# Where the buffers of a fused convolution and two-layer MLP kernel begin: TensorE's streamed operands on 2048-byte boundaries

## The chip, the cores and the metric

The kernel runs on one core of one Trainium2 chip. The time is the device time of one execution in microseconds (us). The kernel before took 1140.1 us, the median of 3 runs (1139.94 to 1140.52).

## What is computed

The input x has 2 sequences of 4096 tokens with 192 channels. Three steps follow, all in float32 in the reference:

```python
# 1. causal convolution: 7 taps, a softmax of 8 heads' weights, 24 channels to a head
out[b, s, h, :] = sum_k w[h, k] * x_pad[b, s + k, h, :]
# 2. a first MLP, 192 -> 2048 -> 192, leaky
h = x @ w_in;  g = np.maximum(0.01 * h, h);  y = g @ w_out
# 3. a second MLP of the same size, smooth
h = y @ w_in2; g = h if h >= 1, 0 if h <= -1, else (h + 1)**2 / 4;  z = g @ w_out2
```

## The kernel before

The 8192 tokens are cut into 16 tiles of T = 512 tokens. Channels lie on the 128 partitions and tokens along the free dimension; the 192 channels are split into a main part of 128 and an edge part of 64. A job is one layer for one tile, so there are 32 jobs; leaky and smooth jobs of neighbouring tiles alternate.

A job goes through CHUNKS = 16 chunks of 128 hidden channels. For each chunk, TensorE makes `hidden` from the tile's operands and the weights w_main and w_edge; ScalarE and VectorE apply the activation and write `g`; the second matmuls add `g` times w_out to `acc_main` and `acc_edge`. To keep float32's precision, each value that TensorE streams is split into a rounded part (`hi`) and the rest (`lo`), both of type fp32r, and so are the weights. ScalarE makes g_hi from g (L682), VectorE makes g_lo = g - g_hi (L951). All streamed operands of the two layers are such buffers of 512 fp32r elements per partition, 2048 bytes: op_hi, op_lo, op_edge and op_top (for both layers, two each: 16 buffers) and g_hi and g_lo (SLOTS = 4 each: 8 buffers).

TensorE's order is written out by hand. Each matmul uses 64 of the array's 128 rows: `top_first` and `top_second` issue for the upper half (partitions 0 to 63), `bottom_first` and `bottom_second` for the lower half. `two_chunks` interleaves them so that one matmul of each half runs beside one of the other: 38 matmuls, 19 for each half, per two chunks. Only the last 20 matmuls (`whole_edge`, `whole_main`) use all 128 rows. In the opening, 16 small matmuls (`keep_warm`, L615) and an edge convolution (L622), both in plain f32, go ahead; the convolution streams 256 elements of x_edge0.

Lines that the prediction speaks of: L411, L413, L415 and L417 are the upper half's matmuls for `hidden`, L429 to L445 the lower half's; L472 to L485 are the upper half's second matmuls, L501 to L513 the lower half's. L522 to L536 are the whole-array ones.

The order in which `sb(...)` is called sets each buffer's address: one buffer is laid behind the other in the partition's memory, each rounded up to 32 bytes. In the kernel before, the weights come first, then the stages for loading weights, ten small buffers for the taps' softmax and `taps`, the x buffers, the op buffers, conv, pre and g, g_hi and g_lo, and the result's buffers. The small tap buffers are written and read once, in the opening.

Of the kernel before, what the change touches and what calls it, by code (L numbers as in the profile page):

```python
# [9 lines left out]

# [1 line left out]

# [4 lines left out]
F32R = mybir.dt.float32r  # L19
# [3 lines left out]

P = 128
T = 512
Q = 32
GROUPS = T // Q
AHEAD = 3
# [4 lines left out]
SLOTS = 4  # L33
# [14 lines left out]
def bass_conv_mlp_mlp(nc, x, weight, moe_w_in, moe_w_out, moe2_w_in, moe2_w_out, out):  # L48
    B, S, D = x.shape
    H, TAPS = weight.shape  # L50
    F = moe_w_in.shape[1]
    GROUP = D // H
    HALO = TAPS - 1
    EDGE = D - P
    CHUNKS = F // P
    HALF = T // 2
    TILES = B * S // T
    STORES = D // Q
    LOADS = P // Q
    assert LOADS == 2 * EDGE // Q  # L60
    PIECES = 8
    PC = CHUNKS // PIECES
    PW = PC * P
# [3 lines left out]

    x_rows = x.rearrange("b s d -> (b s) d").rearrange("(g r) d -> r g d", r=Q)
    out_rows = out.rearrange("(g r) d -> r g d", r=Q)
    w_in_dram = (moe_w_in, moe2_w_in)  # L70
    w_out_dram = tuple(w.rearrange("(c p) d -> p c d", p=P) for w in (moe_w_out, moe2_w_out))

    with ExitStack() as ctx:
        def sb(name, shape, dt=F32):
            return ctx.enter_context(nc.sbuf_tensor(name, shape, dt))

        def psum(name):
            return ctx.enter_context(nc.psum_tensor(name, [P, T], F32))

# [5 lines left out]
        w_main = [sb(f"w_main{l}", [P, 2, F], F32R) for l in (0, 1)]  # L85
        w_edge = [sb(f"w_edge{l}", [P, 2, F], F32R) for l in (0, 1)]
        w_out = [sb(f"w_out{l}", [P, CHUNKS, 2 * D], F32R) for l in (0, 1)]

        stage = [sb(f"stage{i}", [P, 2 * PW + PC * D]) for i in range(AHEAD)]

        taps_raw = sb("taps_raw", [P, H, TAPS])
        taps_max = sb("taps_max", [P, H])
        taps_sub = sb("taps_sub", [P, H, TAPS])
        taps_exp = sb("taps_exp", [P, H, TAPS])
        taps_sum = sb("taps_sum", [P, H])
        taps_den = sb("taps_den", [P, H])
        taps_inv = sb("taps_inv", [P, H])
        own = sb("own", [P, 3, H])
        own_inv = sb("own_inv", [P, 2, H])
        own_taps = sb("own_taps", [P, 2, H, TAPS])  # L100
        taps = sb("taps", [P, 2, TAPS])

        x_in = [sb(f"x_in{b}", [P, T]) for b in (0, 1)]
        x_in_edge = [sb(f"x_in_edge{b}", [P, HALF]) for b in (0, 1)]
        x_main = [sb(f"x_main{b}", [P, HALO + T]) for b in (0, 1)]
        x_edge = [sb(f"x_edge{b}", [P, HALO + HALF]) for b in (0, 1)]

        op_hi = [[sb(f"op_hi{l}{b}", [P, T], F32R) for b in (0, 1)] for l in (0, 1)]
        op_lo = [[sb(f"op_lo{l}{b}", [P, T], F32R) for b in (0, 1)] for l in (0, 1)]
        op_edge = [[sb(f"op_edge{l}{b}", [P, T], F32R) for b in (0, 1)] for l in (0, 1)]
        op_top = [[sb(f"op_top{l}{b}", [P, T], F32R) for b in (0, 1)] for l in (0, 1)]
        conv_main = sb("conv_main", [P, T])
        conv_edge = sb("conv_edge", [P, HALF])

        pre = [sb(f"pre{i}", [P, T]) for i in (0, 1)]
        g = [sb(f"g{i}", [P, T]) for i in range(SLOTS)]
        g_hi = [sb(f"g_hi{i}", [P, T], F32R) for i in range(SLOTS)]  # L120
        g_lo = [sb(f"g_lo{i}", [P, T], F32R) for i in range(SLOTS)]

        edge_b = sb("edge_b", [EDGE, T])
        edge_sum = sb("edge_sum", [EDGE, T])
        y_main = sb("y_main", [P, T])
        y_edge = sb("y_edge", [EDGE, T])

        hidden = [psum(f"hidden{i}") for i in range(SLOTS)]
        acc_main = [psum(f"acc_main{i}") for i in (0, 1)]
# [986 lines left out]
```

How the kernel before makes its waits and increments, by code:

```python
        @block.sync  # L273
# [29 lines left out]
            def store(t, b, pos):  # L303
                group = b * (S // Q) + pos * GROUPS
                sp.wait_ge(y_main_ready, t + 1)
                for q in range(D // Q):
                    if q == P // Q:
                        sp.wait_ge(y_edge_ready, t + 1)
                    src = y_main[Q * q:Q * (q + 1), :] if q < P // Q else y_edge[Q * q - P:Q * (q + 1) - P, :]
                    sp.dma_start(out_rows[:, bass.ds(group, GROUPS), Q * q:Q * (q + 1)],
                                 src.rearrange("r (g c) -> r g c", c=Q)).then_inc(stored, 16)
            load_x_main(EVEN, 0, parts=P // Q - 1)
            load_x_edge(EVEN, 0, parts=range(2))
            load_weights(1)
            load_x_main(ODD, 0)
            load_weights(2)
            load_x_edge(ODD, 0)
            for piece in range(AHEAD, 2 * PIECES):
                sp.wait_ge(stage_used, piece - AHEAD + 1)
                load_weights(piece)
                if piece == PIECES:
                    sp.wait_ge(x_turned, 2)
                    load_x(EVEN, 1)
            with sp.Fori(0, PASSES) as j:
                sp.wait_ge(x_turned, 4 * j + 4)
                load_x(ODD, j + 1)
                store(2 * j, EVEN, j)
                sp.wait_ge(x_turned, 4 * j + 6)
# [1 line left out]
                store(2 * j + 1, ODD, j)  # L331
            store(TILES - 2, EVEN, TILES // 2 - 1)
            sp.wait_ge(y_edge_ready, TILES)
            for q in range(P // Q, D // Q):
```

## Time and profile before

| | before |
|---|---|
| median of 3 runs | 1140.1 us |
| profiled execution's own time | 1139.77 us |
| its span, first to last instruction | 1138.0 us |
| PE busy | 1126.9 us (99%), 9754 matmuls |
| VectorE (DVE) busy | 897.3 us (79%) |
| ScalarE (ACT) busy | 797.8 us (70%) |
| mean granted TensorE clock | 0.999 of full speed |

The span is the time between the first and the last instruction of the profiled execution; the device time is slightly longer. "Busy" of an engine is the time covered by at least one of its instructions; PE is the matmuls and PEld the weight loads, which run beside them. A matmul's duration in the profile is modelled and longer than its distance to the next one, because matmuls overlap in the array; the distance between starts is what can be counted on.

### The profile page before, as it was taken

Reading aid. Unit: us, or ns where it says so; the run is one execution under the profiler, and the core shown is the slowest. Engines: PE = TensorE matmul, PEld = TensorE weight load, DVE = VectorE, ACT = ScalarE, POOL = GpSimd, SP = SyncE. Lnnn points to the kernel's source line nnn. Section 1 sums busy time; section 2 is a strip of 40 time slices with the busy share of each in tenths; the row PEclk is TensorE's granted clock in tenths of the full one; section 3 lists DMA queues with packets and bytes.
Section 4 is the critical chain, followed back from the end, with each engine's and each line's share of the span. In section 5 each row is a group of like instructions: output and inputs, shape, how many; then the busy total and the mean of one; then the engine's idle time right before and its main releaser. Section 6 shows DMA issues by size and latency. Waiting matters only on the chain.

```text
span 1138.0 us, 25723 instructions
## 1 busy us (share of the span) xinstructions
PE 1126.9 (99%) x9754; PEld 922.7 (81%) x9754; DVE 897.3 (79%) x1511; ACT 797.8 (70%) x1472; POOL 50.3 (4%) x76
## 2 busy tenths in 40 slices
PE   7999999999999999999999999999999999999998
PEld 6788888888888888888888888888888888888886
DVE  7787877888777887788877788787787877888665
ACT  6768767586775867758577685866758667686685
POOL 5533000000000000000000000000000000000000
PEclk9999999999999999999999999999999999999999
DMA  6330000101001010010100101001010100100001
GB/s 142 97 80 2 14 16 1 29 2 25 5 1 30 1 29 1 1 29 1 29 1 8 23 1 29 1 13 18 1 29 1 24 7 1 29 1 15 1 1 28
DMA packets 114569, 21.98 MB, mean 19 GB/s; under 512 B 106257, under 2 KB 114449, under 8 KB 114449
## 3 DMA queue, kind: packets, MB, share of 16 engines
q1 hardware_dynamic: 111600, 19.61, 9.4%
q8 instruction: 77, 1.26, 0.5%
q10 hardware_dynamic: 2848, 0.75, 0.3%
q14 instruction: 44, 0.35, 0.1%
HBM read 14.05 MB, written 6.29 MB: 18 GB/s over the span
## 4 chain that ended last, share of the span: by engine, by line
PE 93%; DVE 3%; ACT 2%; issue 1%; DMA 0%; DVEq 0%; ACTq 0%
PE hidden L417 14%; PE acc_edge L475 10%; PE acc_main L481 10%; PE acc_main L483 10%; PE acc_main L485 10%; PE hidden L413 10%; PE hidden L415 10%; PE hidden L411 10%; PE acc_edge L472 10%; DVE g_lo L951 1%; DVE g L940 0%; ACT g_hi L682 0%; DVE acc_main L887 0%; ACT pre L670 0%; DVE acc_main L851 0%
## 5 line engine op out<-in xcount | busy, mean ns | idle before, releaser
L682 ACT CAST g_hi<-g 128x512 fp32r<-128x512 f32 x510 | 299.2, 618 | 280.2 <-PE acc_main L513 214.4
L951 DVE TENSOR_TENSOR g_lo<-g,g_hi 128x512 fp32r<-128x512 f32 x510 | 335.0, 690 | 104.1 <-ACT g_hi L682 99.3
L945 DVE SCALAR_TENSOR_TENSOR g<-hidden,pre 128x512 f32<-128x512 f32 x256 | 176.7, 690 | 105.9 <-ACT pre L670 100.5
L417 PE MATMUL hidden<-op_edge,w_edge 64*128 64x512 f32 x768 | 257.3, 388 | 0.0
L411 PE MATMUL hidden<-op_hi,w_main 64*128 64x512 f32 x512 | 198.9, 389 | 3.2 <-DVE g L940 1.7
L429 PE MATMUL hidden<-op_hi,w_main 64*128 64x512 f32 x512 | 199.2, 389 | 0.0
L433 PE MATMUL hidden<-op_hi,w_main 64*128 64x512 f32 x512 | 198.9, 388 | 0.0
L413 PE MATMUL hidden<-op_lo,w_main 64*128 64x512 f32 x512 | 198.8, 388 | 0.0
L438 PE MATMUL hidden<-op_edge,w_edge 64*128 64x512 f32 x512 | 198.7, 388 | 0.0
L431 PE MATMUL hidden<-op_lo,w_main 64*128 64x512 f32 x512 | 198.7, 388 | 0.0
L415 PE MATMUL hidden<-op_hi,w_main 64*128 64x512 f32 x512 | 198.7, 388 | 0.0
L475 PE MATMUL acc_edge<-g_lo,w_out 64*128 64x512 f32 x508 | 197.6, 389 | 0.5 <-DVE g_lo L951 0.5
L501 PE MATMUL acc_edge<-g_hi,w_out 64*128 64x512 f32 x508 | 197.2, 388 | 0.0
L472 PE MATMUL acc_edge<-g_hi,w_out 64*128 64x512 f32 x508 | 197.1, 388 | 0.0
L509 PE MATMUL acc_main<-g_hi,w_out 64*128 64x512 f32 x508 | 197.1, 388 | 0.0
L513 PE MATMUL acc_main<-g_lo,w_out 64*128 64x512 f32 x508 | 197.1, 388 | 0.0
L481 PE MATMUL acc_main<-g_hi,w_out 64*128 64x512 f32 x508 | 197.1, 388 | 0.0
L485 PE MATMUL acc_main<-g_lo,w_out 64*128 64x512 f32 x508 | 197.1, 388 | 0.0
L511 PE MATMUL acc_main<-g_hi,w_out 64*128 64x512 f32 x508 | 197.1, 388 | 0.0
L483 PE MATMUL acc_main<-g_hi,w_out 64*128 64x512 f32 x508 | 197.1, 388 | 0.0
L503 PE MATMUL acc_edge<-g_lo,w_out 64*128 64x512 f32 x508 | 197.1, 388 | 0.0
L940 DVE SCALAR_TENSOR_TENSOR g<-hidden,pre 128x512 f32<-128x512 f32 x256 | 172.5, 680 | 17.5 <-ACT pre L663 13.9
(128 smaller groups left out, 2778.2 us busy)
## 6 DMA issues: line engine op xcount, KB each, us to landing
x_in<-in_x_dram SPq DMA_DIRECT2D x67, 64.0 KB, 2.3
out_dram<-y_main SPq DMA_DIRECT2D x62, 64.0 KB, 1.8
stage<-in_moe_w_out_dram SPq DMA_DIRECT2D x15, 192.0 KB, 2.7
x_in_edge<-in_x_dram SPq DMA_DIRECT2D x66, 32.0 KB, 1.9
out_dram<-y_edge SPq DMA_DIRECT2D x32, 64.0 KB, 1.8
stage<-in_moe_w_in_dram SPq DMA_DIRECT2D x15, 128.0 KB, 2.3
stage<-in_moe_w_in_dram SPq DMA_DIRECT2D x30, 64.0 KB, 2.3
stage<-in_moe_w_out_dram ACTq DMA_DIRECT2D x1, 192.0 KB, 4.0
```

The lines of the kernel that those rows point to most:

```text
L411: nc.tensor.matmul(h[:], w_main[l][top, 0, cols], op_hi[l][b][top, :], start=True, stop=False)
L413: nc.tensor.matmul(h[:], w_main[l][top, 0, cols], op_lo[l][b][top, :], start=False, stop=False)
L415: nc.tensor.matmul(h[:], w_main[l][top, 1, cols], op_hi[l][b][top, :], start=False, stop=False)
L417: done = nc.tensor.matmul(h[:], w_edge[l][top, i - 3, cols], op_edge[l][b][top, :], start=False, stop=False)
L429: nc.tensor.matmul(h[:], w_main[l][bottom, 0, cols], op_hi[l][b][bottom, :], start=False, stop=False)
L472: nc.tensor.matmul(edge[:], w[:, P:2 * P], hi, start=k == 0, stop=False)
L475: done = nc.tensor.matmul(edge[:], w[:, P:2 * P], lo, start=False, stop=False)
L481: nc.tensor.matmul(main[:], w[:, 0:P], hi, start=k == 0, stop=False)
L483: nc.tensor.matmul(main[:], w[:, 2 * P:], hi, start=False, stop=False)
L485: done = nc.tensor.matmul(main[:], w[:, 0:P], lo, start=False, stop=False)
L682: nc.scalar.copy(hi_of(n, c)[:], g[c % SLOTS][:]).then_inc(g_hi_ready, 1)
L951: nc.vector.tensor_tensor(lo_of(n, c)[:], g[c % SLOTS][:], hi_of(n, c)[:].bitcast(F32), ALU.subtract).then_inc(g_lo_ready, 1)
```

## The change

The order of the buffers is altered, and a filler is put in. Weights stay where they are. Behind them come `taps`, x_edge0 and the filler `to_line`, whose size is computed from the first free byte (16,512) and the weights' 114,688 bytes, so that the op buffers, g_hi and g_lo begin on multiples of 2048 bytes. Stages and x buffers move behind them. The ten small tap buffers are no longer buffers of their own: they are parts of y_main. The instructions, their order, the semaphores and the waits are the same.

```diff
+LINE = 2048
+FIRST_FREE = 16512
...
-        stage = [sb(f"stage{i}", [P, 2 * PW + PC * D]) for i in range(AHEAD)]
-        taps_raw = sb("taps_raw", [P, H, TAPS])
-        taps_max = sb("taps_max", [P, H])
...
         taps = sb("taps", [P, 2, TAPS])
-        x_in = [sb(f"x_in{b}", [P, T]) for b in (0, 1)]
-        x_in_edge = [sb(f"x_in_edge{b}", [P, HALF]) for b in (0, 1)]
-        x_main = [sb(f"x_main{b}", [P, HALO + T]) for b in (0, 1)]
-        x_edge = [sb(f"x_edge{b}", [P, HALO + HALF]) for b in (0, 1)]
+        x_edge = [sb("x_edge0", [P, HALO + HALF])]
+        sb("to_line", [P, (LINE - (FIRST_FREE + 114688) % LINE - 64 - 1056) // 4])
         op_hi = [[sb(f"op_hi{l}{b}", [P, T], F32R) for b in (0, 1)] for l in (0, 1)]
         op_lo = [[sb(f"op_lo{l}{b}", [P, T], F32R) for b in (0, 1)] for l in (0, 1)]
         op_edge = [[sb(f"op_edge{l}{b}", [P, T], F32R) for b in (0, 1)] for l in (0, 1)]
         op_top = [[sb(f"op_top{l}{b}", [P, T], F32R) for b in (0, 1)] for l in (0, 1)]
+        g_hi = [sb(f"g_hi{i}", [P, T], F32R) for i in range(SLOTS)]
+        g_lo = [sb(f"g_lo{i}", [P, T], F32R) for i in range(SLOTS)]
+        x_edge.append(sb("x_edge1", [P, HALO + HALF]))
+        stage = [sb(f"stage{i}", [P, 2 * PW + PC * D]) for i in range(AHEAD)]
+        x_in = [sb(f"x_in{b}", [P, T]) for b in (0, 1)]
+        x_in_edge = [sb(f"x_in_edge{b}", [P, HALF]) for b in (0, 1)]
+        x_main = [sb(f"x_main{b}", [P, HALO + T]) for b in (0, 1)]
         conv_main = sb("conv_main", [P, T])
         conv_edge = sb("conv_edge", [P, HALF])
         pre = [sb(f"pre{i}", [P, T]) for i in (0, 1)]
         g = [sb(f"g{i}", [P, T]) for i in range(SLOTS)]
-        g_hi = [sb(f"g_hi{i}", [P, T], F32R) for i in range(SLOTS)]
-        g_lo = [sb(f"g_lo{i}", [P, T], F32R) for i in range(SLOTS)]
...
         y_main = sb("y_main", [P, T])
         y_edge = sb("y_edge", [EDGE, T])
+        used = 0
+        def in_y_main(*shape):
+            nonlocal used
+            first, used = used, used + math.prod(shape)
+            part = y_main[:, first:used]
...
+        taps_raw = in_y_main(H, TAPS)
+        taps_max = in_y_main(H)
...
+        own_taps = in_y_main(2, H, TAPS)
```

## Rows read from the trace of the kernel before

**Rows 1.** The page, part 1: busy time, share of the span, number of instructions.

```profile
PE 1126.9 (99%) x9754; PEld 922.7 (81%) x9754; DVE 897.3 (79%) x1511; ACT 797.8 (70%) x1472; POOL 50.3 (4%) x76
```

**Rows 2.** The page, part 4: the chain that ended last, by engine.

```profile
PE 93%; DVE 3%; ACT 2%; issue 1%; DMA 0%; DVEq 0%; ACTq 0%
```

**Rows 3.** Stages: window, its length, busy time (instructions) by engine, clock, DMA share.

```profile
0.00:13.40 13.40, 9.39 (x46) 8.48 (x46) 8.20 (x22) 6.73 (x18) 4.60 (x17) 1.00 0.83 164
...
60.00:1128.00 1068.00, 1067.95 (x9323) 875.03 (x9320) 846.90 (x1423) 754.81 (x1377) 18.62 (x24) 1.00 0.08 14
1128.00:1138.00 10.00, 5.20 (x22) 3.68 (x20) 3.68 (x6) 1.32 (x3) 0.00 (x0) 0.89 0.27 39
```

**Rows 4.** Waits of PE, longest in total first: total us, times, longest.

```profile
PE hidden L411 <- DVE g L940: 1.7, 2, 1.5
```

**Rows 5.** Timeline of PE, 500 to 506 us: start us, length us, instruction.

```profile
500.18 0.39 PE L411 MATMUL hidden<-op_hi,w_main 64*128 64x512 f32 x1
...
501.32 0.39 PE L411 MATMUL hidden<-op_hi,w_main 64*128 64x512 f32 x1
...
502.01 0.39 PE L417 MATMUL hidden<-op_edge,w_edge 64*128 64x512 f32 x1
502.01 0.39 PE L429 MATMUL hidden<-op_hi,w_main 64*128 64x512 f32 x1
502.24 0.39 PE L472 MATMUL acc_edge<-g_hi,w_out 64*128 64x512 f32 x1
...
504.07 0.39 PE L483 MATMUL acc_main<-g_hi,w_out 64*128 64x512 f32 x1
504.07 0.39 PE L501 MATMUL acc_edge<-g_hi,w_out 64*128 64x512 f32 x1
504.30 0.39 PE L485 MATMUL acc_main<-g_lo,w_out 64*128 64x512 f32 x1
...
504.53 0.39 PE L411 MATMUL hidden<-op_hi,w_main 64*128 64x512 f32 x1
504.53 0.39 PE L501 MATMUL acc_edge<-g_hi,w_out 64*128 64x512 f32 x1
504.76 0.39 PE L413 MATMUL hidden<-op_lo,w_main 64*128 64x512 f32 x1
...
505.67 0.39 PE L411 MATMUL hidden<-op_hi,w_main 64*128 64x512 f32 x1
```

**Rows 6.** Timeline of PE at the end, whole-array matmuls.

```profile
1130.98 0.39 PE L533 MATMUL acc_main<-g_hi,w_out 128*128 128x512 f32 x1
...
1131.66 0.39 PE L533 MATMUL acc_main<-op_hi,w_out 128*128 128x512 f32 x1
...
1132.35 0.39 PE L533 MATMUL acc_main<-op_hi,w_out 128*128 128x512 f32 x1
```

**Rows 7.** Timeline of PE at the edge convolution, whole and its first two records.

```profile
8.72 3.29 PE L622 MATMUL acc_edge<-x_edge,g 128*128 128x256 f32 x14 [1.50 <-ACT x_edge L655]
...
8.72 0.70 PE L622 MATMUL acc_edge<-x_edge,g 128*128 128x256 f32 x2 [1.50 <-ACT x_edge L655]
```

**Rows 8.** Timeline of PE in the opening of job 0.

```profile
13.45 0.50 PE L411 MATMUL hidden<-op_hi,w_main 64*128 64x512 f32 x1 [1.44 <-ACT op_hi L709]
...
15.53 0.39 PE L431 MATMUL hidden<-op_lo,w_main 64*128 64x512 f32 x1
...
17.62 0.39 PE L431 MATMUL hidden<-op_lo,w_main 64*128 64x512 f32 x1
```

**Rows 9.** Two successive jobs in the middle, columns as in rows 3.

```profile
504.00:539.00 35.00, 35.00 (x310) 28.69 (x308) 27.33 (x50) 28.63 (x51) 0.00 (x0) 1.00 0.01 2
539.00:574.00 35.00, 35.00 (x310) 28.69 (x308) 28.28 (x46) 20.24 (x39) 0.00 (x0) 1.00 0.15 24
```

**Rows 10.** The chain in order of time, opening: start us, length us, what.

```profile
0.81 3.18 DMA taps_raw<-in_weight_dram
...
6.00 0.35 DVE taps L1072
```

**Rows 11.** Timeline of the weight loads at 500 us.

```profile
500.18 0.18 PEld L413 LDWEIGHTS hidden<-op_lo,w_main 64*128 64x128 f32 x1
```

More of the change, by code:

```diff
@@ L13 @@
+import math
 from contextlib import ExitStack
@@ L87, in bass_conv_mlp_mlp @@
         w_out = [sb(f"w_out{l}", [P, CHUNKS, 2 * D], F32R) for l in (0, 1)]
-        stage = [sb(f"stage{i}", [P, 2 * PW + PC * D]) for i in range(AHEAD)]
-        taps_raw = sb("taps_raw", [P, H, TAPS])
-        taps_max = sb("taps_max", [P, H])
[L93 to L100, printed above, removed]
         taps = sb("taps", [P, 2, TAPS])
-        x_in = [sb(f"x_in{b}", [P, T]) for b in (0, 1)]
-        x_in_edge = [sb(f"x_in_edge{b}", [P, HALF]) for b in (0, 1)]
-        x_main = [sb(f"x_main{b}", [P, HALO + T]) for b in (0, 1)]
-        x_edge = [sb(f"x_edge{b}", [P, HALO + HALF]) for b in (0, 1)]
+        x_edge = [sb("x_edge0", [P, HALO + HALF])]
+        sb("to_line", [P, (LINE - (FIRST_FREE + 114688) % LINE - 64 - 1056) // 4])
         op_hi = [[sb(f"op_hi{l}{b}", [P, T], F32R) for b in (0, 1)] for l in (0, 1)]
@@ L126, in bass_conv_mlp_mlp @@
         y_edge = sb("y_edge", [EDGE, T])
+        used = 0
[3 more added lines that the diff above has]
+            part = y_main[:, first:used]
+            if len(shape) == 1:
+                return part
+            if len(shape) == 2:
+                return part.rearrange("p (a b) -> p a b", b=shape[1])
+            return part.rearrange("p (a b c) -> p a b c", b=shape[1], c=shape[2])
+        taps_raw = in_y_main(H, TAPS)
+        taps_max = in_y_main(H)
+        taps_sub = in_y_main(H, TAPS)
+        taps_exp = in_y_main(H, TAPS)
+        taps_sum = in_y_main(H)
+        taps_den = in_y_main(H)
+        taps_inv = in_y_main(H)
+        own = in_y_main(3, H)
+        own_inv = in_y_main(2, H)
+        own_taps = in_y_main(2, H, TAPS)
         hidden = [psum(f"hidden{i}") for i in range(SLOTS)]
```

## The prediction

> **What bounds the kernel now.** I read the page's busy shares first, then the chain, then a table by stage, then single starts on TensorE. The busy shares put PE at 99% and no other engine above 81% [rows 1]. The chain gives PE 93% of the span and leaves at most 7% to all other causes together [rows 2]. The table by stage shows where the 7% lies: from 60 to 1128 us PE is busy 1067.95 of 1068.00 us, so that all of its idle time is in the opening and in the last 10 us [rows 3]. The list of PE's waits agrees: its longest total is 1.7 us [rows 4]. In 94% of the span nobody keeps TensorE waiting, and only the distance between two of its starts counts.
>
> That distance is read in the timeline. Two matmuls start together, one on the array's upper 64 rows and one on the lower 64, and the next two follow. L411 at 500.18 and L411 at 504.53 are two chunks, or 19 such pairs, apart: 4.35 us / 19 = 228.9 ns [rows 5]. The table by stage confirms it over the whole stretch: 9323 records / 2 in 1068 us is 229.1 ns, with a few records missing [rows 3]. The granted clock there is 1.00, which is 2.4 GHz, and 512 columns at one a cycle are 213.3 ns. So each start carries 15.5 ns more than its columns.
>
> How many starts are there? 32 jobs of 8 units of two chunks, 19 pairs each: 4,864, and 20 whole-array matmuls at the end. Together some 4,884. One nanosecond per start is 4.9 us of span. That is the whole lever of this change.
>
> **Where the streamed operands lie.** The allocator lays the buffers out in the order of the code, each rounded up to 32 bytes, from byte 16,512 (the constant that the change itself writes down). Before: 16,512 + 114,688 (weights) + 10,752 (three stages) + 1,472 (tap scraps) + 4,096 + 2,048 + 4,160 + 2,112 (x buffers) = 155,840, which is 76 x 2048 + 192. All sixteen op buffers are 2,048 long and so all lie at 192. The first g_hi is 48,128 further, at 203,968 = 99 x 2048 + 1,216; all g_hi and g_lo lie at 1,216. After: 131,200 + 64 (taps) + 1,056 (x_edge0) + 800 (filler) = 133,120 = 65 x 2048, and op, g_hi and g_lo follow without a gap, all at 0. Each is a stream of exactly 2,048 bytes per partition: before it ran over one boundary, after it runs over none. A weight block (512 bytes) of w_main lies at 128, 640, 1,152 or 1,664 by chunk, before and after; the last of these runs over a boundary.
>
> **Part 1: the streams move from 192 or 1,216 to 0.** Nothing of the trace has a stream at 0, so the price is bounded by what the trace does vary.
> - Which of the two offsets: L417 with L429 at 502.01 are both at 192, L483 with L501 at 504.07 both at 1,216, L411 with L501 at 504.53 one of each. The next start comes 0.23 us behind each [rows 5]. With the whole array too: L533 reads g_hi (1,216) at 1130.98 and op_hi (192) at 1131.66, and the runs of three behind them take 0.68 and 0.69 us [rows 6]. So the offset's place above 1,024 costs nothing, nor whether two halves have the same one. But 192 and 1,216 are the same number modulo 1,024, and both run over one boundary: the trace is silent on exactly what the change alters.
> - Weight blocks: any four successive chunks go through all four places. Consecutive L411 at 500.18, 501.32, 504.53 and 505.67 keep the same rhythm of 1.14 and 3.21 us [rows 5]; the block that runs over a boundary costs nothing seen.
> - Lower bound on time: the nearest row without the surplus is the edge convolution, L622. Its first record lies at 8.72, its second starts at 8.72 + 0.70 - 0.38 = 9.04 and its fourteenth at 8.72 + 3.29 - 0.38 = 11.63 [rows 7]: 2.59 us / 12 = 216 ns for 256 columns in two passes, also 512 cycles. If the boundary is what costs, the change gains 228.9 - 216 = 12.9 ns per start, 12.9 x 4,884 = 63 us.
> - Upper bound on time: the widest steps without a wait are in the opening, where the halves run half a step apart: L431 at 15.53 to L431 at 17.62 is 9 starts, 232.2 ns [rows 8]. That is 3.3 ns more, 3.3 x 4,884 = +16 us.
> - I take 0 ns, the value nearest to the rows that do vary an offset, and keep both ends.
>
> A rule of the Trainium skill bears on this, in "Advanced Engine Details and Errata", section "Memory Cachelines": SBUF has lines of 16 bytes, and an access that goes to another line pays. 192 and 1,216 are multiples of 16 already, so by this rule a start at 0 crosses the same 128 lines and the sum stays at zero. The steps of [rows 5] agree as far as they reach.
>
> **Part 2: the rest of the layout.** Stages, x_in, g and pre now begin 32 bytes off a multiple of 64, where they were on one. ScalarE and VectorE read and write them, and the DMAs fill stage and x_in. In the middle of the kernel two successive jobs (two more repeat them) leave VectorE 27.3 to 28.3 of 35 us busy and ScalarE 20.2 to 28.6 [rows 9], and PE waits for neither, so a few per cent more on them stays covered; without that cover 1% of VectorE's 897 us would be 9 us. The one exposed place is the opening, where the taps' transfer of 3.18 us and VectorE's chain behind it are on the path [rows 10]. Ten nanoseconds on each of 30 such pieces are 0.3 us either way.
>
> **Part 3: the tap scraps share y_main.** They are written and read before 6.4 us [rows 10]; y_main's first transpose comes in job 3, and a job is 8 x 4.35 = 34.8 us long. The taps themselves have a buffer of their own. No instruction, semaphore or wait is added. Cost 0.
>
> **Sum.** 0 ns x 4,884, 0 and 0: span 1138.0 us. The profiled execution took 1139.77 us, 1.8 more than its span, and lies 0.3 below the median of 1140.1. I forecast 1140.1 us for the median, and for this case alone 1138.5 to 1141.7.
>
> **Rivals.**
> *The boundary is the surplus.* Each fp32r stream of the kernel runs over one boundary and pays 12.9 ns; streams that do not, L622's, pay nothing. For it: the change alters exactly this, and no row contradicts it. Against it: two places of crossing, 832 and 1,856 bytes into the stream, cost the same, which is natural for a crossing but as natural for a constant of fp32r, and L622 differs in its type too. Time: 1140.1 - 63 = 1077 us. What would then be late is not VectorE: 28.3 busy of 35 would be 28.3 of 33. The Trainium skill speaks on the size, in "TensorE: Matmul & The Clock Gate", section "Wait — 56ns, not 53.3ns?": a warm matmul follows the last after N / 2.4 GHz plus about 2.5 ns, with no term for type or address; an estimate from it is 215.8 ns and 1076 us. L622's 216 ns agree, the 228.9 of the fp32r streams do not, so something that this rule leaves out is at work here.
>
> *The crossing is a part of it.* Half of the 12.9 ns goes: 6.4 x 4,884 = 31 us, 1109 us. Only the sense of the first speaks for it.
>
> *The streams fall into step with the weight loads.* Each load begins with the stream of the same partitions (L413's load at 500.18 beside L411's matmul at 500.18) and takes 184 ns of its 229 [rows 5, 11]. If both are served from places chosen by the low part of the address, the distance between them matters: before 64 bytes modulo 512 (192 - 128), after 128 bytes the other way. All chunks would meet more often, at every start, and the place to see it is the plain rhythm. Its price is the widest step seen, 232.2 ns: 1140.1 + 16 = 1156 us; it decides from 0.5 ns per start on, which is 2.3 us. For it: the rhythm does stretch when the halves' phase shifts [rows 8]. Against it: that stretch is at the kernel's opening, with transfers and GpSimd at work, and moving weights by 512 bytes costs nothing [rows 5].
>
> **Numbers.** No effect (or addresses that don't come out as worked out, which reads the same) 0.55; the whole surplus 0.18; a part 0.07; in step 0.20. A measurement of this kernel tells 0.2%, 2.3 us, from no change. Faster 0.25, same 0.55, slower 0.20. The range reaches to the prices of the first and last rival, 1075 to 1157; beyond it lie only slower cases with a price above the widest step seen, some 0.05.
>
> **What would show it.** In the profile after, the distance of two L411 that are two chunks apart: 4.35 us if I am right, 4.10 if the boundary was the surplus, 4.23 for a part, 4.41 or more for the rival in step. PE's 1068 us of full business must stay full; if PE shows waits for VectorE or ScalarE in the middle, part 2 was mis-sized. The opening must end, with L411's first start, within 0.3 us of 13.45 [rows 8]. A span off by over 2.3 us at an unchanged 228.9 ns would make the whole working wrong, for I know no other lever of that size.

## The result

| | before | after |
|---|---|---|
| median device time | 1140.24 us (5 runs) | 1156.22 us (6 runs) |
| span of the profiled execution | 1138.0 us | 1154.1 us |
| PE busy | 1126.9 us | 1143.3 us |
| VectorE, ScalarE busy | 897.3, 797.8 us | 897.3, 798.3 us |
| mean granted clock | 0.999 | 0.999 |

A sixth run of the kernel before took 5722.32 us and is left out. The five others took 1139.94 to 1140.52 us, the six of the changed kernel 1155.84 to 1160.55. The ratio of after to before is 1.0146, 95% interval [1.0129, 1.0162] (of the medians, 1.0140): the change makes the kernel 16 us slower. The forecast, no effect, was wrong.

First the table by stage of the changed kernel, columns as in [rows 3].

```profile
0.00:13.40 13.40, 9.34 (x46) 8.43 (x46) 8.20 (x22) 6.73 (x18) 4.42 (x17) 1.00 0.85 163
...
60.00:1128.00 1068.00, 1068.00 (x9194) 864.80 (x9192) 836.25 (x1407) 742.59 (x1355) 18.72 (x24) 1.00 0.08 13
```

PE is busy without a break as before, at the same clock, but fits 9194 matmul records into the 1068 us where it fitted 9323 [rows 3]: 9323 / 9194 = 1.0140, which is the ratio of the medians, 1156.22 / 1140.24, and so the whole slowdown. The timeline of PE (start, length, instruction; L423 is the line that was L411) shows the same in single starts:

```profile
502.24 0.39 PE L423 MATMUL hidden<-op_hi,w_main 64*128 64x512 f32 x1
...
503.39 0.40 PE L423 MATMUL hidden<-op_hi,w_main 64*128 64x512 f32 x1
...
506.64 0.40 PE L423 MATMUL hidden<-op_hi,w_main 64*128 64x512 f32 x1
...
507.81 0.39 PE L423 MATMUL hidden<-op_hi,w_main 64*128 64x512 f32 x1
```

Two chunks now take 4.40 to 4.42 us (502.24 to 506.64, 503.39 to 507.81) instead of 4.35 [rows 5], 232 ns per start instead of 228.9. The opening and the end are untouched. In PE's timeline there:

```profile
13.45 0.49 PE L423 MATMUL hidden<-op_hi,w_main 64*128 64x512 f32 x1 [1.43 <-ACT op_hi L721]
...
1148.91 0.40 PE L548 MATMUL acc_main<-op_lo,w_out 128*128 128x512 f32 x1
```

The first start is at 13.45 as in [rows 8]; the last is at 1148.91. In the kernel before, the last was at 1132.81:

```profile
1132.81 0.39 PE L536 MATMUL acc_main<-op_lo,w_out 128*128 128x512 f32 x1
```

The last start comes 16.1 us later, which is the whole difference of the spans: 16.1 / 4,884 = 3.3 ns per start. The longest waits of PE are still some 1.5 us each, in the opening; the one of [rows 4] now reads (total us, times, longest):

```profile
PE hidden L423 <- DVE g L952: 1.5, 1, 1.5
```

The single steps have a pattern that the mean hides. Differences of successive starts around 500 us, in ns:

```
before: 232 226 229 | 231 226 229 | 232 226 229 | 232 226 229 | 231 226 229 ...
after:  241 232 231 232 228 230 233 | 241 232 231 232 228 230 232 | 241 233 231 231 229 230 232 ...
```

Before, three starts repeat; after, seven, and one of them takes 241 ns. This goes on across chunks and jobs, whatever matmul is next. So the step does not depend on the matmul alone; something carried over from one start to the next seems to decide it.

### The profile page after: what moved, and what is told of

Its sections match the earlier page's. It is cut to its first block, busy times and chain, and to the rows that moved or that the text cites. A ratio compares the mean times of both kernels' runs of the same rounds, so it can differ in the third digit from the quotient of the medians.

```text
span 1154.1 us, 25723 instructions
## 1 busy us (share of the span) xinstructions
PE 1143.3 (99%) x9754; PEld 925.6 (80%) x9754; DVE 897.3 (78%) x1511; ACT 798.3 (69%) x1472; POOL 50.2 (4%) x76
## 4 chain that ended last, share of the span: by engine, by line
PE 96%; DVE 3%; ACT 1%; issue 0%; DMA 0%; DVEq 0%
PE hidden L429 15%; PE acc_edge L487 10%; PE acc_main L497 10%; PE acc_main L495 10%; PE acc_main L493 10%; PE hidden L423 10%; PE hidden L425 10%; PE hidden L427 10%; PE acc_edge L484 10%; DVE g L952 0%; DVE g_lo L963 0%; DVE acc_main L899 0%; DVE acc_main L863 0%; DMA y_main<-in_weight_dram 0%; PE acc_main L525 0%
## 5 line engine op out<-in xcount | busy, mean ns | idle before, releaser
L423 PE MATMUL hidden<-op_hi,w_main 64*128 64x512 f32 x512 | 200.6, 392 | 2.9 <-DVE g L952 1.5
```

Of the source, the lines that this page charges most:

```text
L423: nc.tensor.matmul(h[:], w_main[l][top, 0, cols], op_hi[l][b][top, :], start=True, stop=False)
```

## The experiments

Theory A: the absolute place of the streams sets the step (a start on a boundary is bad). Theory B: the distance in bytes from the weights to the streams, modulo some small number, sets it, because the stream and the weight load that runs beside it are read from the same partitions at the same time. Theory C: something else of the new layout costs it.

**1. Undo only the streams' place.** The changed layout with 192 bytes more filler:

```diff
-        sb("to_line", [P, (LINE - (FIRST_FREE + 114688) % LINE - 64 - 1056) // 4])
+        sb("to_line", [P, 992 // 4])
```

> The changed layout with 192 bytes more filler ahead of the op buffers: all streams begin 192 bytes behind a 2048-byte boundary (g_hi and g_lo too, which lay at 1,216 before), weights at 128, everything behind the streams 192 bytes further, the tap scraps still in y_main. Theory A (the absolute place of the streams sets TensorE's step) and theory B (their distance from the weights sets it): 4.35 us for two chunks, 228.9 ns per start, about 1140 us. Theory C (something else of the new layout costs it: stages, g and pre 32 bytes off a multiple of 64, scraps in y_main): 4.41 us, 232.4 ns, 1156 us.

Measured: 1140.07 us against 1139.96 for before in the same rounds, ratio 1.0002 [0.9992, 1.0011]. Theory C is out: stages, g and pre 32 bytes off a multiple of 64 and scraps in y_main cost nothing. And g_hi and g_lo at 192 are as good as at 1,216.

**2. Move the weights to a boundary too** (a filler of 1,920 bytes ahead of the weights, none between weights and streams; taps and x_edge0 go behind g_lo).

```diff
+        sb("ahead", [P, 1920 // 4])
         w_main = [sb(f"w_main{l}", [P, 2, F], F32R) for l in (0, 1)]
```

> Weights moved to a 2048-byte boundary as well, streams stay on one (distance 0 instead of 128 bytes). Theory A (absolute place of the streams): unchanged at 232.4 ns per start, 1156 us. Theory B (distance between streams and weights): another step than 232.4 ns; if nearer is worse, above it, 1160 us or more. Theory C: stage, g and pre are on multiples of 64 here, so 228.9 ns if that was the cost.

Measured: 1129.46 us in a single run, below both kernels. The streams lie at the same addresses as in the changed kernel; of what TensorE reads in the middle, the weights alone were moved. Theory A falls here. Theory B's guess that nearer is worse was wrong: distance 0 is the fastest so far.

**3. Move weights and streams together by 64 bytes** (the same filler line with 64 bytes, the rest as in the change).

> The changed layout moved up by 64 bytes as a whole, weights included: streams at 64, weights at 192, distance 128 as in the changed kernel, and each stream runs over a boundary again. Theory A: the step returns to 228.9 ns, 1140 us (if only a start on a boundary is bad). Theory B and theory C: 232.4 ns, 1156 us.

Measured: 1156.06 us in a single run. No stream begins on a boundary and each runs over one, and the time is that of the changed kernel.

**4. Streams at 0, the old distance of 64 bytes** (1,856 bytes ahead of the weights, only `taps` between them and the streams).

> Streams at 0 as in the changed kernel, weights at 1,984, so that the streams are 64 bytes ahead of the weights modulo 2048, as the op buffers were in the kernel before. Theory A: 232.4 ns, 1156 us. Theory B: 228.9 ns, 1140 us. Theory C: stage, g and pre are on multiples of 64, 228.9 ns.

Measured: 1139.38 us in a single run. The streams lie at 0 and run over no boundary, and the time is that of the kernel before. With 3 this settles it in both directions: the distance counts, the boundary doesn't.

**5. The function by itself.** One kernel in which TensorE runs 44 segments after each other. A segment is one line, such as

```python
for i in range(29): nc.tensor.matmul(ps[2][:, 0:512], w[:, 0:128], x[:, 16:528], start=True, stop=True)  # distance 64
```

> No part of the convolution or the layers is computed: constants are written to the output, and TensorE runs 44 segments of 29 whole-array matmuls, each with its own weight load, with the place of the weights (w) and of the 512 streamed fp32r columns (s) modulo 2048 as the only difference. Theory B (only the distance s - w counts, through reads of the stream and of the weight load that meet): 226.7 ns per start at distance 0, 229.0 at 64, 232.4 at 384 (that is 128 the other way, modulo 512); w 64 with s 64 as distance 0; w 64 with s 0 as 448; distances of 512, 1,024 and 1,536 as 0; streams of 128 to 384 columns lose less per start, bf16 streams (2 bytes a column) lose little or nothing, under 217 ns. Theory A2 (each operand's own place counts): w 64 with s 64 differs from 0 with 0, and w 128 with s 192 from distance 64.

PE's timeline, merged by line: start, length, instruction, count. A step is the distance from one segment's start to the next, over 29. L53 is distance 0, L54 4 bytes, L59 64, L63 128, L68 256, L69 320, L70 384, L71 448, L92 384 columns at distance 0, L93 384 columns at distance 384, L95 bf16 at distance 0.

```profile
29.11 6.74 PE L53 MATMUL ps<-x,w 128*128 128x512 f32 x29
35.68 7.02 PE L54 MATMUL ps<-x,w 128*128 128x512 f32 x29
42.54 6.93 PE L55 MATMUL ps<-x,w 128*128 128x512 f32 x29
...
69.54 6.80 PE L59 MATMUL ps<-x,w 128*128 128x512 f32 x29
76.18 6.86 PE L60 MATMUL ps<-x,w 128*128 128x512 f32 x29
...
96.33 6.92 PE L63 MATMUL ps<-x,w 128*128 128x512 f32 x29
103.09 6.93 PE L64 MATMUL ps<-x,w 128*128 128x512 f32 x29
...
130.18 6.74 PE L68 MATMUL ps<-x,w 128*128 128x512 f32 x29
136.75 6.82 PE L69 MATMUL ps<-x,w 128*128 128x512 f32 x29
143.41 6.90 PE L70 MATMUL ps<-x,w 128*128 128x512 f32 x29
150.15 6.93 PE L71 MATMUL ps<-x,w 128*128 128x512 f32 x29
...
276.53 5.19 PE L92 MATMUL ps<-x,w 128*128 128x384 f32 x29
281.57 5.27 PE L93 MATMUL ps<-x,w 128*128 128x384 f32 x29
...
299.19 6.42 PE L95 MATMUL ps<-xb,wb 128*128 128x512 bf16 x29
305.45 6.42 PE L96 MATMUL ps<-xb,wb 128*128 128x512 bf16 x29
```

Read off: 6.57 us / 29 = 227 ns at distance 0, 6.86 / 29 = 237 at 4 bytes, 229 at 64, 233 at 128, 227 at 256, 230 at 320, 232 at 384. The single starts give it more sharply (mean without the first of a segment, ns; where a segment takes some starts to settle, they are in the mean):

| distance, bytes | 0 | 4 | 8 | 16 | 32 | 64 | 96 | 128 | 160 | 192 | 224 | 256 | 320 | 384 | 448 |
|---|---|---|---|---|---|---|---|---|---|---|---|---|---|---|---|
| step, ns | 226.7 | 236.6 | 233.3 | 231.8 | 233.0 | 228.9 | 233.1 | 233.5 | 234.1 | 233.3 | 233.2 | 226.7 | 229.3 | 232.0 | 233.2 |

Distances of 512, 1,024 and 1,536 gave 226.7 to 226.9, and w 64 with s 0 gave 233.3 like 192 and 448. w 64 with s 64 began at 224 to 236 and settled at 226.7 within some ten starts, w 128 with s 192 settled at 228.9 the same way. So theory B held and A2 fell. Shorter streams lost less, as expected: between distances 0 and 384, 384 columns took 173.3 and 175.9 ns, 256 columns 120.0 and 119.0 once settled, and 128 columns 111.7 at either, over twice their 53.3, so that something else sets the step there. bf16 streams took 215.9 ns at distance 0 and at 384; plain f32 ones took 215.8 at 0, and in the run of experiment 10 also at 384. Of the three types only fp32r shows the effect, as far as these two distances tell.

**6. The kernel before, with one filler of 192 bytes.** This is the prediction of the function for a layout in which neither weights nor streams lie on a boundary.

```diff
         taps = sb("taps", [P, 2, TAPS])
+        sb("shift", [P, 192 // 4])
```

> The kernel before with one filler of 192 bytes behind the tap buffers and nothing else: weights stay at 128, the op buffers go from 192 to 384, g_hi and g_lo from 1,216 to 1,408, so that the distance streams - weights is 256 modulo 512 for all. Theory B with the function measured alone (226.7 ns per start at 256): 2.2 ns less per start, 10.8 us, about 1129.3 us. Rival (a fast step needs an operand on a 2048-byte boundary, as the streams and weights of the fastest layout so far had): no operand is on one here, so 1140 us or more.

Measured: 1129.17 us (before in the same rounds 1140.28), ratio 0.9903 [0.9886, 0.9919], 0.1 us from what the function gave. Its timeline (L412 is L411 moved by the added line):

```profile
500.43 0.39 PE L412 MATMUL hidden<-op_hi,w_main 64*128 64x512 f32 x1
...
504.73 0.39 PE L412 MATMUL hidden<-op_hi,w_main 64*128 64x512 f32 x1
...
509.04 0.39 PE L412 MATMUL hidden<-op_hi,w_main 64*128 64x512 f32 x1
```

Four chunks take 8.61 us, so two take 4.305 us, 226.6 ns per start.

**7. The same with 128 bytes**, a distance that the function calls bad.

> The kernel before with a filler of 128 bytes in the same place: distance 192 for the op buffers and 192 modulo 512 (1,216 + 128 - 128) for g_hi and g_lo. Theory B with the function measured alone (233.3 ns at 192): 4.4 ns more per start, 21 us, about 1161 us. Rival (own places): nothing that lay on a boundary is moved, 1140 us.

Measured: 1160.27 us in a single run. Its timeline:

```profile
504.03 0.39 PE L412 MATMUL hidden<-op_hi,w_main 64*128 64x512 f32 x1
...
508.46 0.40 PE L412 MATMUL hidden<-op_hi,w_main 64*128 64x512 f32 x1
```

4.43 us / 19 = 233.2 ns. Between this and experiment 6, 64 bytes of filler are 31 us.

**8. Experiment 2 again**, four runs instead of one.

> Weights and streams both on 2048-byte boundaries, timed in rounds: about 1129.4 us as in the single look, the same as the kernel before with 192 bytes of filler, if only the distance modulo 256 counts; faster than it, if a boundary gives something of its own.

Measured: 1129.64 us, ratio 0.9906 [0.9889, 0.9922], not to be told from experiment 6. Boundaries give nothing of their own.

**9. The changed kernel, with the streams alone moved by another 128 bytes** (filler of 928 bytes), to the weights' own place modulo 2048.

> The changed kernel with 128 bytes more filler ahead of the op buffers: streams at 128, where the weights are, distance 0 modulo 2048, each stream over one boundary again. Theory B: 226.7 ns per start, 5.7 ns less than the changed kernel, 28 us, about 1128.5 to 1129.5 us. Rival (the move off the boundary only takes back the loss): 1140 us.

Measured: 1130.08 us, ratio to before 0.9914 [0.9898, 0.9931]. The upper end of what was expected (1129.5) was missed by 0.6 us.

All the layouts together; w, s and the distance s - w are in bytes, the step is the mean of the single steps between 60 and 1120 us of the trace:

| kernel | w | s | distance modulo 256 | step, ns | device time, us |
|---|---|---|---|---|---|
| experiment 6 | 128 | 384, 1,408 | 0 | 226.7 | 1129.17 |
| experiments 2, 8 | 0 | 0 | 0 | 226.7 | 1129.46, 1129.64 |
| experiment 9 | 128 | 128 | 0 | 226.7 | 1130.08 |
| before | 128 | 192, 1,216 | 64 | 228.9 | 1140.24 |
| experiment 1 | 128 | 192 | 64 | 228.9 | 1140.07 |
| experiment 4 | 1,984 | 0 | 64 | 228.9 | 1139.38 |
| after | 128 | 0 | 128 | 232.4 | 1156.22 |
| experiment 3 | 192 | 64 | 128 | 232.4 | 1156.06 |
| experiment 7 | 128 | 320, 1,344 | 192 | 233.3 | 1160.27 |

Runs of one kernel differ by up to 4.7 us here (the changed kernel's 1155.84 to 1160.55), and 1129.46, 1139.38, 1156.06 and 1160.27 are single runs. The steps don't scatter like that: layouts of one distance agree within 0.1 ns.

**10. Is the rest of the surplus the weight load's?** At the best distance 512 columns still take 226.7 ns, 13.3 more than their 213.3, and 384 columns 173.3, again 13.3 more than their 160.

> Again no part of the model is computed; segments of 29 fp32r matmuls of 512 columns with weight loads of 32, 64, 96 and 128 columns (128, 256, 384 and 512 bytes per partition), single and paired 64-row halves, and further distances. Theory M (a weight load takes read slots from the stream of the same partitions, one array cycle per 16 bytes of weights even at the best distance): 512 columns are 213.3 ns, and the surplus at distance 0 is proportional to the width, 13.3 ns at 128, 6.7 at 64 (220.0 ns), 3.3 at 32 (216.7). Rival F (fp32r streams have a fixed cost per start): 226.7 ns at every width. Halves: a pair with distances 0 and 384 goes at the step of the worse (232.4 ns) if the two wait for each other, each at its own if not.

PE's timeline, read as in 5. L53 is a load of 32 columns, L56 of 64, L59 of 96, all at distance 0; L57 is a load of 64 columns at distance 64, L66 distance 20, L80 distance 492, L81 distance 500.

```profile
28.30 6.88 PE L53 MATMUL ps<-x,w 128*32 128x512 f32 x29
35.02 6.89 PE L54 MATMUL ps<-x,w 128*32 128x512 f32 x29
...
48.44 6.83 PE L56 MATMUL ps<-x,w 128*64 128x512 f32 x29
55.11 6.78 PE L57 MATMUL ps<-x,w 128*64 128x512 f32 x29
61.73 6.82 PE L58 MATMUL ps<-x,w 128*64 128x512 f32 x29
...
68.39 6.84 PE L59 MATMUL ps<-x,w 128*96 128x512 f32 x29
75.06 6.92 PE L60 MATMUL ps<-x,w 128*96 128x512 f32 x29
...
115.18 7.12 PE L66 MATMUL ps<-x,w 128*128 128x512 f32 x29
122.13 6.93 PE L67 MATMUL ps<-x,w 128*128 128x512 f32 x29
...
210.02 6.74 PE L80 MATMUL ps<-x,w 128*128 128x512 f32 x29
216.59 7.12 PE L81 MATMUL ps<-x,w 128*128 128x512 f32 x29
223.55 6.83 PE L82 MATMUL ps<-x,w 128*128 128x512 f32 x29
```

Both were wrong. 32 columns of weights took 231.7 ns, 64 took 230.0, 96 took 230.1: not the 216.7 and 220.0 of theory M, and not rival F's 226.7 at every width either. A shorter load does not give the stream its time back. Nor is distance 0 the best for every load: with 64 columns of weights, distance 64 took 228.4 ns against 230.0 at distance 0, and with 32 columns, distance 384 took 230.4 against 231.7. Of the further distances the worst were 20 and 500 bytes with 240.0 ns. Some that are no multiple of 256 settled at 226.7 too: 252 and 492 here, 496 and 508 in experiment 5. None of some forty places settled below 226.7.

The paired halves of these segments started apart, and the single starts tell each half's step. The lag is the time by which one half starts behind the other. In the two pairs of distances 0 and 384, one half settled at 226.7 ns, the step of distance 0, and the other at 232.4 or 233.3, steps that distance 384 has alone, while their lag changed by some 100 ns: neither waited for the other. In the pair of 64 and 64 one half went at 228.9 and the other at 233.3.

The pair of 0 and 0 shows one thing more. In the other pairs the load of each half begins 2 to 4 ns behind the start of its own stream. Here, from the third start on, the loads of both halves began 1 to 6 ns behind the starts of one half, and so 5 to 134 ns behind those of the other. The first half went at 226.7 ns, the other unevenly at 227 to 240, some 233 in the mean. At one and the same distance, then, a stream whose load begins later goes with another step. It is one segment, and it was not made for this.

**11. Phase and start.**

> No part of the model is computed; segments of 42 fp32r matmuls of 512 columns, each behind a short pause, so that no segment inherits its phase from the one before. Theory P (the step depends on the distance modulo 256, and on the phase between stream and weight load, which settles into a repeating pattern): 64 and 320 both 229.0 ns, 192 and 448 both 233.3, 4 and 260 modulo 256 both 236.6; where 240 and 496 (236.5 and 226.7 ns before) or 128 and 384 (233.5 and 232.0) still differ, the period is 512 and not 256; if they agree, only the phase at the start had differed. Paired 64-row halves of distance 0 that start together stay together at 226.7 ns; with the lower half late by 64 to 448 columns each half takes more, 232 to 241 ns, until the two fall into step. Rival: halves don't touch each other, 226.7 ns whatever the lag.

Behind a pause, 64 and 320 took the pattern of three (228.9), 128 and 384 the pattern of seven (232.4), 192 and 448 gave 233.3 to 233.5, 240 and 496 both 236.5: the period is 256 in these four pairs. Distance 4 (236.7) agrees with 260 in experiment 10 (236.7), and eight more pairs of experiments 5 and 10 agree within 0.3 ns. One pair did not agree: 20 bytes gave 240.0 and 276 gave 236.0. Behind six starts at distance 0, however, 240 and 496 both went at 233.3 and 384 at 233.5, and in experiment 5, behind 480, 496 had gone at 226.7. Distance 64 has a second pattern too, the 233.3 of the paired halves. So a distance can hold more than one repeating pattern and the start picks it. Distance 0, behind six starts at 384, was back at 226.7 from its second start on; every single stream at distance 0 fell into the fast pattern.

Halves that start together at distance 0 stay 3 to 4 ns apart at 226.7 ns. In the late pairs the edit delays the upper half, not the lower as the expectation has it. At distance 0 with a lag of 64 to 448 columns, the lag changes for up to ten starts, then holds, and both halves go at 226.7 ns. Their first steps (231, 236, 228, 233, 231 ns, say) are those of a whole-array stream behind a pause at distance 0, where no second half runs beside it. So they are each stream's own way into its pattern. At distance 64 with a lag of 384 columns the lag kept on drifting, because one half went at 228.9 ns and the other at 233.3. With distances 0 and 384 one half went at 226.7 ns and the other at 233.3, each in its pattern, while the lag grew from under 10 ns to some 200. The rival held: in this run no half slows the other. What theory P had right of the halves is only that the steps are longer at first.

## Why the prediction was wrong

The view of what bounds the kernel was right, and so was the lever: nothing but the distance between starts changed, times 4,884. Parts 2 and 3 were right: the same layout with the streams 192 bytes on came back to 1.0002 of before, the opening ended at 13.45, and PE got no new wait.

The step that failed is in part 1: "I take 0 ns, the value nearest to the rows that do vary an offset". This term of the sum measured 3.3 ns per start (16.1 us over 4,884 starts), as much as the upper bound. In its place the runs showed that the step follows the distance from weights to streams modulo 256, which the change took from 64 to 128. The rows that varied an offset varied it by 1,024 (192 against 1,216) and by 512 (the weight blocks), which are whole periods of 256. The prediction said that "the trace is silent on exactly what the change alters", and then let these rows vote all the same. They were no evidence for zero: they tested one point of the function again and again. Nor was the distance from the weights to the streams a term of the sum, though the addresses that give it stood in the text; it came up only in the third rival. (A slip on which nothing rests: 228.9 less 213.3 is a surplus of 15.6 ns, not 15.5.)

That rival, "the streams fall into step with the weight loads", named the mechanism, the two distances (64 against 128 the other way) and the time, 1156 us, and got 0.20. That the distance decides is what the experiments showed, modulo 256 and not 512; that both are served from the same places stays argued. Its price was luck. The 232.2 ns of [rows 8] are the lower half's alone, in its first starts behind a wait, at the old distance. The upper half went at its usual step in the same stretch:

```profile
15.44 0.39 PE L415 MATMUL hidden<-op_hi,w_main 64*128 64x512 f32 x1
...
17.50 0.39 PE L415 MATMUL hidden<-op_hi,w_main 64*128 64x512 f32 x1
```

That is 2.06 us for 9 starts, 228.9 ns. The 232.4 of the changed kernel come from the pattern of seven at the new distance. The objection against the rival, "moving weights by 512 bytes costs nothing", was the same mistake once more. That "all chunks would meet more often" is said too much: how often reads meet was not seen, only the step.

The first two rivals fell: with streams that run over no boundary the kernel took 1156.22 us (after), 1139.38 us (experiment 4) and 1129.46 us (experiment 2), and L622's 216 ns are those of the plain f32 streams of experiments 5 and 10 (215.8).

The 16-byte rule of the Trainium skill ("Advanced Engine Details and Errata", "Memory Cachelines") was used to support the zero; all of the kernels' places are multiples of 16 and they differ by 31 us, so the rule does not cover this. Another rule speaks on the very point: "TensorE: Matmul & The Clock Gate", section "Step-by-step: what each phase is for", gives TensorE one read port for the stream and another for the weights and says that loading weights doesn't take read bandwidth from the running matmul. For the bf16 segments the runs agree (215.9 ns at distances 0 and 384). For fp32r the measurement decides otherwise: with the streams at the same addresses, moving the weights changed the time from 1156.22 to 1129.46 us, which a load that leaves the stream alone would not.

What stays open: what in the chip meets there. The distance from the load's place to the stream's sets the step, with a period of 256 bytes in all pairs but one (20 and 276), and that is shown. That both queue for the same piece of memory is argued; the uneven half of experiment 10, whose loads began late, speaks for a meeting of the two reads. Why one distance can hold several patterns is not known. A stream without any weight load beside it was not tried, so whether the last 13.3 ns at distance 0 belong to the load is not known; the widths of experiment 10 speak against a simple share of it.

## What to carry to other kernels

Where TensorE streams fp32r without a break, look at the address of the weights and of the streams modulo 256: for weight loads of 128 columns make the distance 0, by a filler if need be. For narrower loads try other distances, since 64 columns went faster at 64 than at 0. Here 192 bytes gained 1.0% over the kernel before, and 128 bytes cost 1.8%. Any change that adds or moves a buffer shifts this distance unseen, so compare the distance between matmul starts before blaming the change itself. And when rows are used to bound an effect of an address, ask by which multiples they vary it: rows that all lie one period apart are one row.

## What the runs showed of the hardware that was not expected

- An fp32r stream of 512 columns beside a weight load of 128 columns takes 226.7 to 240.0 ns at a granted clock of 1.00, by the distance and, at some distances, by what ran ahead; bf16 (512 columns) and plain f32 (256 columns) take 215.8 to 215.9 at the two distances tried.
- The steps fall into exact repeating patterns: 226, 227, 227 at distance 0; 226, 229, 232 at 64; seven steps with one of 241 at 128; a constant 240 at 20 bytes. Distance 496 went at 226.7, 233.3 or 236.5, by what ran ahead.
- The best distance still leaves 13.3 ns per start, the same for 256, 384 and 512 columns, and at distance 0 narrower weight loads (32 to 96 columns) make the step longer, 230.0 to 231.7 ns, not shorter.
- Two 64-row halves with distances 0 and 384 go at different steps side by side, 226.7 and some 233 ns, and the lag between them drifts: neither half slows the other there.
- Plain fillers in the right place did the same as boundaries of 2048 bytes; the 2048-byte boundary itself changed nothing: streams that begin on it and streams that run over it took 1156.22 and 1156.06 us at distance 128, 1139.38 and 1140.07 us at distance 64.
